# Expert routing on one core: a tally from four wide products, and products and halves moved within a routing step

## The reference

```python
attn_out = _attn_ref(...)            # (4, 8, 768, 64): chunked attention
x = attn_out as (N=3072, D=512)
# layer one: every token goes to one of E=8 experts, each takes cap=384 tokens
logits = x @ w_gate
for idx in argsort(-logits.flatten()):     # best pair of token and expert first
    tok, e = idx // E, idx % E
    if assigned[tok] >= 0 or counts[e] >= cap: continue
    assigned[tok] = e; counts[e] += 1
for e in range(E):
    out[assigned == e] = np.maximum(x[assigned == e] @ w1[e], 0.0) @ w2[e]
# layer two: two experts of eight for each token, weighted, with noise on the gate
```

## Time and profile before

| what | value |
|---|---|
| three runs, median (lowest to highest) | 1332.58 us (1332.58 to 1336.51) |
| the profiled execution, its own time | 1322.12 us |
| its span | 1320.4 us |
| mean granted clock of TensorE | 0.968 |
| busy: TensorE, VectorE, ScalarE, GpSimd | 1229.1, 916.9, 574.0, 287.1 us |
| routing steps 0 and 1 | about 200 to 285 us |
| routing steps 2 to 6 | about 285 to 542 us |

### The profile page before, as it was taken

How to read it: one execution, slowest core, us unless ns; L and a number is a source line. 1 busy time by engine, 2 the same in 40 slices (tenths; PEclk the granted TensorE clock), 3 DMA queues, 4 the chain that set the end, 5 groups by cost and what they waited for, 6 DMA issues and landing times.

```text
span 1320.4 us, 27840 instructions
## 1 busy us (share of the span) xinstructions
PE 1229.1 (93%) x9680; PEld 1093.4 (83%) x9680; DVE 916.9 (69%) x1826; ACT 574.0 (43%) x1232; POOL 287.1 (22%) x346
## 2 busy tenths in 40 slices
PE   6999983289999999999999999999999999999997
PEld 5888872277787787888898999989999899999986
DVE  4777765897887887765696666667666666666662
ACT  4666650123333233344415544545455444544541
POOL 4000000202202102120214332423233242332422
PEclk9999995589999999999999999999999999999999
DMA  8788744433332432543315233233434423334210
GB/s 147 168 169 167 165 99 176 153 112 106 128 121 64 149 127 75 177 150 121 110 34 192 66 110 112 80 104 103 128 119 127 141 79 104 100 125 135 88 43 13
DMA packets 174298, 154.65 MB, mean 117 GB/s; under 512 B 105117, under 2 KB 137885, under 8 KB 174240
## 3 DMA queue, kind: packets, MB, share of 16 engines
q1 hardware_dynamic: 151552, 102.83, 27.9%
q0 software_dynamic: 16128, 44.56, 11.1%
q10 hardware_dynamic: 6560, 6.49, 1.4%
HBM read 206.13 MB, written 33.75 MB: 182 GB/s over the span
## 4 chain that ended last, share of the span: by engine, by line
issue 37%; PE 36%; DVE 10%; POOL 9%; DMA 4%; ACT 2%; POOLq 1%; DVEq 0%; ACTq 0%
PE bank L766 8%; PE bank L786 6%; DMA out<-result,token_now 3%; PE bank L642 3%; POOL partial L421 3%; POOL out L431 3%; PE bank L651 2%; PE bank L630 2%; POOL held L401 2%; PE bank L666 2%; PE bank L1000 2%; POOL x L405 2%; PE bank L712 2%; PE bank L1027 2%; PE bank L751 1%
## 5 line engine op out<-in xcount | busy, mean ns | idle before, releaser
L569 DVE TENSOR_TENSOR w_part<-w_sb,w_part 128x1024 fp32r<-128x1024 f32 x280 | 341.7, 1224 | 104.2 <-ACT w_part L563 96.7
L563 ACT CAST w_part<-w_sb 128x1024 fp32r<-128x1024 f32 x280 | 290.5, 1046 | 206.8 <-PE bank L1027 154.4
L1000 PEld LDWEIGHTS bank<-x2T,w_part 128*128 128x128 f32 x2688 | 326.3, 192 | 3.7 <-issue 1.0
L1000 PE MATMUL bank<-x2T,w_part 128*128 128x256 f32 x2688 | 328.0, 283 | 1.1 <-DVE x2T L1557 0.6
L1027 PE MATMUL bank<-w_part,h2T 128*128 128x512 f32 x1344 | 312.6, 391 | 0.0
L1027 PEld LDWEIGHTS bank<-w_part,h2T 128*128 128x128 f32 x1344 | 250.1, 188 | 51.0
L786 PE MATMUL bank<-w_part,hT 128*128 128x512 f32 x576 | 154.9, 406 | 3.7 <-DVE w_part L569 3.7
L766 PE MATMUL bank<-xgT,w_part 128*128 128x384 f32 x768 | 146.4, 343 | 1.2 <-DVE xgT L1221 1.2
L1915 ACT ACTIVATE h2T<-bank 128x512 fp32r<-128x512 f32 x112 | 66.9, 597 | 176.8 <-PE bank L1000 176.8
L379 POOL DMA_INDIRECT xg<-x_dram,token_of x24 | 29.5, 1230 | 510.1 <-DVE token_of L1256 269.2
L766 PEld LDWEIGHTS bank<-xgT,w_part 128*128 128x128 f32 x768 | 133.6, 190 | 2.9 <-DVE xgT L1221 1.4
(11 more groups left out here) (281 smaller groups left out, 1306.7 us busy)
## 6 DMA issues: line engine op xcount, KB each, us to landing
w_sb<-in_moe_w SPq DMA_DIRECT2D x280, 512.0 KB
k_in<-in_k SPq DMA_DIRECT2D x32, 240.0 KB
v_in<-in_v SPq DMA_DIRECT2D x32, 240.0 KB
q_in<-in_q SPq DMA_DIRECT2D x32, 192.0 KB
x_dram<-x_sb SPq DMA_DIRECT2D x32, 192.0 KB, 3.0
out<-zeros SPq DMA_DIRECT2D x1, 6144.0 KB, 19.7
y_dram<-y_sb ACTq DMA_DIRECT2D x24, 256.0 KB, 2.0
x<-y_dram,slot_now POOLq DMA_INDIRECT x56, 3.6
```

The costliest lines, as they stand in the source:

```text
L563: scalar.copy(split_part(0, c), raw_part(c)).then_inc(hi_ready[c], 1)
L569: nc.vector.tensor_tensor(split_part(1, c), raw_part(c), split_part(0, c).bitcast(F32), ALU.subtract).then_inc(lo_ready[c], 1)
L1000: last = nc.tensor.matmul(bank[2 + g % 2][:, at:at + TILE], w1_part[a][:, kt, f * P:(f + 1) * P], x2T[b][:, kt, :], start=(f % 2 == 0 and ...
```

## The change

The tally, 24 products of the `ones` matrix with 16 columns each, which added up in PSUM, becomes four products with 96 columns each (six token columns by 16). The six partial sums per value that are left in PSUM are added by VectorE, in a reduction that takes the place of the copy. The region of the ranks in the bank moves up to make room; the votes stay at column 32, which is `BINS`.

On TensorE `gate_y(j, 1)` goes from between the seventh count and its vote to behind the vote and the combine pieces after it; `gate_y(j, 2)` goes from behind `hidden(k, 1)` to ahead of the wait for the tied tokens. On ScalarE `copy_gate(j, 1)` goes behind `xg_high(k, 3)` and `w_high(k, 4)`, and stays ahead of `copy_y(j, 2)`; `copy_gate(j, 2)` goes ahead of `w_high(k, 5)` and `s1_high(k, 1)`. On VectorE `s1_low(k, 3)` goes ahead of `w_low(k, 5)`, the last two pieces of a step.

```diff
--- before.py
+++ after.py
@@ -50,6 +50,7 @@
     SLOTS = TILES * TILE // P
     ROW = DM + 2 * E
     CH = 4
+    TALLY = 6
     NT = B * BLOCKS
     assert F == 1024 and CAP * E == N and TPE == 3 and E == 8 and TILES % 2 == 0 and EARLY_TILES == 2
 
@@ -701,8 +702,8 @@
 
 
 
-            counts, votes_ps, tally_ps, ranks_ps = (bank[7][0:BINS, 0:E], bank[7][:, BINS:BINS + E], bank[7][:, 64:64 + 2 * E],
-                                                    bank[7][:, 80:80 + 2 * COLS])
+            counts, votes_ps, tally_ps, ranks_ps = (bank[7][0:BINS, 0:E], bank[7][:, 32:32 + E], bank[7][:, 64:64 + 2 * E * TALLY],
+                                                    bank[7][:, 192:192 + 2 * COLS])
 
             def count(n, s):
 
@@ -811,8 +812,6 @@
                         if s == 0:
                             hidden(j, FT - 2)
                         combine(j, done, before_votes[s])
-                        if s == 6:
-                            gate_y(j, 1, k)
                     vote(n, s)
                     if k is not None:
                         if s == 2:
@@ -826,25 +825,24 @@
                         done = after_votes[s]
                         if s in (3, 5):
                             turn_y(j, (s - 3) // 2)
-                        if s == 4:
-                            gate_y(j, 0, k)
+                        if s in (4, 6):
+                            gate_y(j, (s - 4) // 2, k)
                 pe.wait_ge(chosen_up, n + 1)
-                for c in range(COLS):
-                    last = nc.tensor.matmul(tally_ps, ones[:], chosen[:, c, :], start=(c == 0), stop=(c == COLS - 1))
+                for c in range(0, COLS, TALLY):
+                    last = nc.tensor.matmul(tally_ps, ones[:], chosen[:, c:c + TALLY, :].rearrange("p c e -> p (c e)"),
+                                            start=(c == 0), stop=(c + TALLY == COLS))
                 last.then_inc(tally_up, 1)
                 if j is not None:
                     turn_y(j, 2)
                 if k is not None:
                     hidden(k, 0)
+                if j is not None:
+                    gate_y(j, 2, k)
                 pe.wait_ge(tied_up, n + 1)
                 nc.tensor.matmul(ranks_ps[:, 0:COLS], before[:], tied[:], start=True, stop=True)
                 nc.tensor.matmul(ranks_ps[:, COLS:2 * COLS], ones[:], tied[:], start=True, stop=True).then_inc(ranks_up, 1)
                 if k is not None:
-                    hidden(k, 1)
-                if j is not None:
-                    gate_y(j, 2, k)
-                if k is not None:
-                    for f in range(2, 4):
+                    for f in range(1, 4):
                         hidden(k, f)
 
                 if j is not None:
@@ -1413,7 +1411,7 @@
                     w_low(k, CH, 1)
 
                 dve.wait_ge(tally_up, n + 1)
-                link(V.tensor_copy(tally[:], tally_ps))
+                link(V.tensor_reduce(tally[:], tally_ps.rearrange("p (c e) -> p e c", c=TALLY), AX.X, ALU.add))
                 link(V.tensor_tensor(et[0][:], tally[:, 0:E], tally[:, E:2 * E], ALU.add))
                 link(V.tensor_tensor(et[1][:], et[0][:], room[:], ALU.is_ge))
                 link(V.tensor_tensor(et[2][:], et[1][:], order_w[:], ALU.mult))
@@ -1448,8 +1446,8 @@
                 link(V.tensor_reduce(colt[0][:], hot[:], AX.X, ALU.max))
                 link(V.tensor_tensor(free[:], free[:], colt[0][:], ALU.subtract))
                 if k is not None:
+                    s1_low(k, 3)
                     w_low(k, CH + 1, 1)
-                    s1_low(k, 3)
 
             def fill_last():
 
@@ -1813,22 +1811,20 @@
                     copy_yT(j, 1)
                 if k is not None:
                     xg_high(k, 2)
+                    xg_high(k, 3)
+                    w_high(k, CH, 1)
                 if j is not None:
                     copy_gate(j, 1)
-                if k is not None:
-                    xg_high(k, 3)
-                    w_high(k, CH, 1)
                 if j is not None:
                     copy_y(j, 2)
                     copy_yT(j, 2)
                 if k is not None:
                     s1_high(k, 0)
-                    w_high(k, CH + 1, 1)
-                    s1_high(k, 1)
                 if j is not None:
                     copy_gate(j, 2)
                 if k is not None:
-                    for f in range(2, 6):
+                    w_high(k, CH + 1, 1)
+                    for f in range(1, 6):
                         s1_high(k, f)
                     w_high(k, CH + 2, 1)
                     w_high(k, CH + 3, 1)
```

## The result

The changed kernel took 1342.17 us (five runs, 1339.79 to 1343.98), the kernel before 1332.58 beside it: a ratio of 1.0057, 95% interval 1.0043 to 1.0072. That is 9.6 us slower than before, and above the forecast of 1332.7 and its range of 1326.5 to 1337.8. Later chips ran the same changed kernel against before at 1.0030 (1.0018 to 1.0043), 1.0034 (1.0020 to 1.0047) and 1.0044 (1.0002 to 1.0085), and before itself took 1323 us on them. So the change loses 4 to 6 us there and 9.6 in the first measurement: slower each time, by sums that differ.

A forecast was written before the change was run, and what follows sets the result against it. It took TensorE as the busiest engine, idle four times a step in steps 2 to 6, 12.6 us together; -0.2 + 1.05 + 0.1 - 0.87 = +0.1 us on the median gave 1332.7 us, range 1326.5 to 1337.8.

The forecast's parts named there:

- step 0, first count to first count: Step 0, where nothing covers the tally: four wide products and the reduction together give -0.2 us.
- four wide products at the low clock: Step 0's tally on TensorE: 0.5 us taken, between 0.3 and 0.58, against 0.81 for the old tally.
- `hidden(k, 2)` earlier: TensorE, steps 2 to 6: without gate_y of tile 2 behind hidden 1, hidden 2 to 5 come 0.87 us earlier.
- TensorE idle ahead of `turn_y`: Steps 2 to 6: copy_y stands behind copy_gate, so TensorE is idle 0.6 us before turn_y.
- VectorE's wait behind `free`: Steps 2 to 6: VectorE stands idle 1.0 us for the high half of low half 3.
- TensorE idle ahead of the first count: Steps 2 to 6: TensorE's idle time before the next step's count grows from 0.58 to about 1.6 us.
- step 1: hidden 3 isn't earlier there, so VectorE's wait costs 0.97 us and the reduction 0.08, together +1.05 us.
- joints of steps 2 to 6: Four joints between steps 2 and 6: each costs +0.02 us, together +0.1; with no slack 0.5.
- behind step 6: With no count to wait for, the 0.87 us that each step wins stays this once: -0.87.
- the clock among the rivals: Step 1, idle 0.65 us between hidden 0 and 1: clock rises one group later, +1.9 us, 1334.6; chance 0.06.
- The slow rival: VectorE's wait for low half 3 costs 1.05 us at all five joints, exit gives nothing: +5.1, 1337.6; chance 0.13.
- fast rival: Steps 2 to 6: idle time before the ties goes, the tally's 0.48 is kept: gain 6.5 us, 1326.1; chance 0.15.

The follow-up runs named there:

- VectorE's order put back: The changed kernel with `w_low(k, CH + 1, 1)` ahead of `s1_low(k, 3)` again on VectorE: 1320.61 us, 0.9976 of before.
- the changed kernel's second profile: The changed kernel run again on a later chip with no edit: 1326.63 us, 1.0030 of before.
- The filler: The changed kernel with 22 unused 128-column products behind hidden 5 in each step with an expert k: 1325.05 us, 1.0018 of before.
- the two edits on VectorE: The changed kernel with VectorE's old order, 1320.61 us (0.9976); the kernel before with only low half 3 ahead of weight half six, 1332.3 us (1.0069).
- the best version: The changed kernel with VectorE's old order and `copy_y(2)` ahead of `copy_gate(1)` on ScalarE: 1316.83 us, 0.9954 of before.
- the products in step 0: 100 more 8-column products, 20 behind each of five votes of step 0: on the changed kernel 1328.23 us (1.0039), on the best version 1318.43 us (0.9958).

## Why the prediction was wrong

**The mechanics held.** Step by step, the changed kernel against before:

| step of the prediction | forecast, us | measured, us |
|---|---|---|
| step 0, first count to first count | -0.2 | 32.70 to 32.47: -0.23 |
| four wide products at the low clock | 0.5 | 0.50 |
| reduction of 96 | 0.25 | 0.25 |
| `hidden(k, 1)` earlier, before against VectorE's order put back | 0.07 | 0.06 |
| `hidden(k, 2)` earlier, in the same two | 0.87 | 0.89 |
| TensorE idle ahead of `turn_y` | 0.6 | 0.66 to 0.68 |
| VectorE's wait behind `free` | 1.0 | 1.05 |
| TensorE idle ahead of the first count | 1.6 | 1.59 to 1.66 |
| step 1 | +1.05 | 46.66 to 47.61: +0.95 |
| joints of steps 2 to 6, clock held | +0.02 each | 51.49 and 51.50 against 51.50 |
| behind step 6, last first count to the ranks | -0.87 | 69.79 to 68.76: -1.03 |

The measured side is from the changed kernel's second profile and before's first, where the line doesn't say otherwise. The 0.07 us came out although the prediction's own lines don't give it: `gate_y` ends at 427.10 there, 0.11 behind before's ranks at 426.99. The 427.10 is a modelled end, and the product behind it begins earlier.

In the changed kernel's second profile, from the first count to the ranks behind step 6, these make 357.1 us against 355.2: -0.2 + 0.95 - 1.03, and 1.1 twice for the two falls, 1.9 in all.

**The step that failed** is the one that said of the idle time ahead of the count that it "grows from 0.58 to about 1.6 us" and charged for it only by the lateness of the count. The sum put the clock there at nothing, and gave no reason. The longer idle time has a price of its own: behind it the granted clock can fall, and then the 12 products of a hidden group take up to 3.9 us instead of 2.4. Over all 18 profiles, a fall stands behind 21 of the 35 first counts of steps 2 to 6 that had 1.59 to 1.66 us of idle time ahead (seven profiles), and behind none of the 55 that had 0.34 to 0.81 (eleven profiles). Where a step without a fall stands beside it in the same profile, such a fall costs 1.0 to 1.2 us (late signals aside), and the changed kernel has two or three of them in each of those. The filler shows that the idleness brings them, and the two edits on VectorE show that it is that order which makes the idleness.

Not every fall is of this kind: others begin in the sixth round and cost 1.6 to 1.7 us each. The changed kernel's later profiles have none, two, two and one of them. One is in the kernel with the wide tally alone, and one in the best version with the products in step 0 (a period of 51.69 us among three of 49.92 to 49.99), neither with a long idle time ahead. What sets those stays open.

**What the prediction did not look at** is all that lies behind the routing steps, which it let move along unchanged. In the second profile the span is 9.1 us above before's. The start of routing is 0.6 of it, as much by chance as in any pair of these profiles; the steps are 1.9; from the ranks to layer two's first product of a weight part 1.5, with a low stretch in it; and layer two 5.1, with the gather's 1.8 and a low stretch behind it, from 722.4 to 729.2 us. The four profiles of the changed kernel on later chips (one with the products in step 0) have 1.9, 6.1, 6.1 and 3.9 us more in the steps, and 5.1, 4.1, 4.4 and 0.9 in layer two. So the loss of 4 to 6 us lies in both places, in shares that change from run to run, and where it is large the clock has fallen. For layer two all 18 profiles say so: it takes 673.2 to 674.3 us in the three with a low stretch of 6.8 us behind the gather, 671.8 to 671.9 in the three where that stretch is 3.4 us, two of which are versions with VectorE's old order, and 668.7 to 671.2 in the twelve without one. Why the gather is later, and why the clock falls there, stays open: putting back the program's length did not bring the time back, and the moment at which the transfer meets the weight loads was not set by itself.

I had the clock among the rivals, but in step 1 alone, behind the idle time of 0.65 us, at 1334.6 and a chance of 0.06. The idle time there came out at 0.23 to 0.28 us where `hidden(k, 0)` ran at the low clock throughout: the 0.65 is the 0.57 us that the tally saves at the full clock and 0.08 for the reduction, but at the low clock of that step the tally saves 0.31. In no run did the clock rise a whole group later. It did rise somewhat later inside `hidden(k, 1)` in some, with the wide tally (step 1 of 48.10 us in the changed kernel with 100 more products, 47.6 in the others) and with the old one (47.12 with the gate moves alone, 46.89 with `copy_y` ahead). I had put the same question to the small idle time and not to the five large ones that my own sum made. The rule of the Trainium skill that I cited (TensorE: Matmul & The Clock Gate, "What's actually happening": activity releases the throttle) bears on both; the traces agree with it (0.57 on average over the four microseconds behind an idle time of 1.59 us, 1.00 over the same four with the idle time filled).

**The slow rival** (1.05 us in every step) did not happen in the changed kernel, since hidden 3 was 0.9 us earlier, but it is what VectorE's order does to the kernel before: 0.9 us a step. The **fast rival** asked for VectorE not to be in the way and copy_y not to wait; with VectorE's old order and `copy_y` ahead it gives -6.4 us (0.9952), where the prediction had -6.5. That they meet so closely is in part luck: in the profile the stretch from the first count to the ranks is 8.2 us shorter than before's (347.0 against 355.2), and layer two 1.0 longer.

**In the first measurement** there is a further term. By the later ratios the changed kernel would take 1336.6 to 1338.4 us where before takes 1332.58, at the upper end of the range; what carries it on to 1342.17 was not seen again. The late signals cost 1.2 us in a step: the one step there without a fall behind its count takes 52.72 us against 51.50. Five of them are 6 us. The stretch is 371.4 us long against 355.2 in before's profile, 16.2 more: -0.3 for the table's steps, 6 for the late signals, and the remaining 10.5 for falls. Four stretches of low clock begin behind the count (the 12 products take 3.9, 3.6, 3.9 and 3.7 us), and three more in sixth rounds. How much of the falls and late signals before has on that chip was not seen; its median there is 9 to 10 us above that on the others, so part of them at least seems to be in both, which is argued, not shown. The ratio of 1.0057 against 1.003 to 1.004 is not explained beyond that.

The tally was sized right, and so was the forecast that it would gain nothing here.

## What to carry to other kernels

When a reordering trades a short wait of TensorE for a longer one at another place, charge the longer one twice: once for what comes late, and once for the clock, by what the products behind it lose at the low level times the chance that it falls. Here that was 1.1 us and 21 in 35, some 3 us over five steps. A low half put ahead of independent work on an in-order engine pays only if it is ready when the engine comes; look at when its input ends, in every kind of step (here step 1, where nothing had moved forward, lost a whole microsecond). Where two changes of this size are compared, the stretch behind them belongs in the sum as well. And a copy that waits for a product moved back must not stand ahead of one that others wait for: exchanging these two was worth 0.4 to 0.6 us a step.

## What the runs showed of the hardware

The three profiles of before have idle times of 0.4 to 0.8 us, four in a step, and no low clock between 285 and 1310 us; idle times of 1.6 us ahead of the first count brought one in 21 of 35 steps, and not in the others, with the same order and the same idle time. Products of 8 columns followed each of them, so whether idleness of that length alone does it wasn't told apart; before's wait for the gather in layer two, 1.22 to 1.94 us with products of 128 columns behind it, brought none in three profiles. The changed kernel thus spreads over 1323.3 to 1333.3 us from run to run on the later chips, before over 1321 to 1327, and the changed kernel's clock over the run, 0.958 to 0.967, is the lower of the two (0.966 to 0.969 in before).

TensorE's results can reach other engines more than a microsecond behind their modelled end: in the sixth round of five steps, in one profile, `met` began 1.69 to 1.75 us behind the end of its count, where every other profile has 0.04 us in the same places. In step 4 both VectorE and ScalarE began at 423.7 us what was due near 422.0 and 422.5. The kernel before took 1332.58 us beside the first measurement and 1322.7 to 1323.5 on five later chips, 9 to 10 us less; a ratio to before taken beside it stands, a time in microseconds from another chip does not.
